# Weight chunks split between a softmax and its user, output copies moved forward in their slots, and the splits of the next tile's x moved: one edit of an attention and two-FFN kernel

## The reference, cut to what matters

```python
def _attn_ref(q, k, v):                      # 4 batches, 8 heads, 576 positions, 64 wide
    q_d, k_d, v_d = (means over groups of 4 positions)
    out_up = np.repeat(sm_attn(q_d, k_d, v_d), 4, axis=2)
    scores = np.where(abs(i - j) < 4, scale * q @ k.T, -1e9)
    return out_up + softmax(scores) @ v

x = attention.transpose(0, 2, 1, 3).reshape(2304, 512)
h = x @ w_in                                  # 512 -> 2048
x = (np.maximum(h, 0) + alpha * np.minimum(h, 0)) @ w_out
h = x @ w2_in
out = np.where(h > 0, h, np.exp(np.minimum(h, 0)) - 1) @ w2_out
```

## Time and profile before

| | us |
|---|---|
| median of 3 runs | 931.96 (930.35 to 935.31) |
| the profiled execution | 933.14 |
| its span in the trace | 931.3 |
| PE busy | 911.6 (98%) |
| DVE busy | 544.0 (58%) |
| ACT busy | 339.2 (36%) |
| POOL busy | 280.7 (30%) |
| mean granted TensorE clock | 0.993 |

### The profile page before, as it was taken

How to read it: one execution, slowest core, us unless ns; L and a number is a source line. 1 busy time by engine, 2 the same in 40 slices (tenths; PEclk the granted TensorE clock), 3 DMA queues, 4 the chain that set the end, 5 groups by cost and what they waited for, 6 DMA issues and landing times.

```text
span 931.3 us, 15268 instructions
## 1 busy us (share of the span) xinstructions
PE 911.6 (98%) x5616; PEld 851.6 (91%) x5616; DVE 544.0 (58%) x1071; ACT 339.2 (36%) x784; POOL 280.7 (30%) x399
## 2 busy tenths in 40 slices
PE   8797999999999999999999999999999999999998
PEld 6697999999999999999999998888888898888887
DVE  6663566655665555454456475656765657756563
ACT  6762444444443332232232132323442234523233
POOL 3799872111111125554656541110011100000000
PEclk9998999999999999999999999999999999999999
DMA  7655531222111123353444234333453443544411
GB/s 168 147 149 147 129 110 41 54 54 51 49 45 28 29 61 125 122 161 125 159 152 143 68 125 123 113 116 113 124 181 115 115 123 114 170 126 122 115 46 69
DMA packets 119834, 100.70 MB, mean 108 GB/s; under 512 B 66000, under 2 KB 82384, under 8 KB 119760
## 3 DMA queue, kind: packets, MB, share of 16 engines
q1 hardware_dynamic: 118576, 99.42, 37.5%
q10 hardware_dynamic: 1184, 0.30, 0.2%
HBM read 80.29 MB, written 19.40 MB: 107 GB/s over the span
## 4 chain that ended last, share of the span: by engine, by line
PE 88%; POOL 6%; DVE 3%; issue 2%; ACT 1%; DVEq 0%; POOLq 0%; ACTq 0%
PE ps L243 27%; PE ps L245 26%; PE ps L244 26%; PE ps L442 2%; POOL w_in_lo L731 1%; POOL w_out_lo L731 1%; PE ps L486 1%; PE ps L424 1%; POOL w_hi L723 1%; DVE common L300 1%; PE ps L432 1%; PE ps L473 1%; POOL p_l L703 1%; POOL p_c L700 1%; PE ps L457 1%
## 5 line engine op out<-in xcount | busy, mean ns | idle before, releaser
L245 PE MATMUL ps<-common,w_hi 128*128 128x384 f32 x768 | 258.8, 337 | 0.0
L244 PE MATMUL ps<-common,w_hi 128*128 128x384 f32 x768 | 258.6, 337 | 0.0
L244 PEld LDWEIGHTS ps<-common,w_hi 128*128 128x128 f32 x768 | 145.2, 189 | 0.0
L245 PEld LDWEIGHTS ps<-common,w_hi 128*128 128x128 f32 x768 | 144.8, 189 | 0.0
L243 PE MATMUL ps<-common,w_in_lo 128*128 128x384 f32 x384 | 133.9, 349 | 0.4 <-DVE common L300 0.4
L243 PE MATMUL ps<-common,w_out_lo 128*128 128x384 f32 x384 | 132.9, 346 | 0.5 <-DVE common L322 0.5
L318 ACT ACTIVATE common<-act_g 128x384 fp32r<-128x384 f32 x96 | 50.4, 525 | 214.6 <-PE ps L245 125.1
L882 ACT ACTIVATE act_g<-act_g 128x384 f32<-128x384 f32 x96 | 50.5, 526 | 196.0 <-DVE act_g L878 196.0
L243 PE MATMUL ps<-w_hi,common 128*128 128x512 f32 x288 | 113.8, 395 | 1.7 <-ACT xT L331 1.0
L307 DVE TENSOR_SCALAR act_g<-ps,alpha_t 128x384 f32<-128x384 f32 x96 | 59.2, 617 | 95.5 <-PE ps L245 95.3
L245 PE MATMUL ps<-w_hi,common 128*128 128x512 f32 x288 | 113.5, 394 | 0.0
(11 more groups left out here) (104 smaller groups left out, 1537.2 us busy)
## 6 DMA issues: line engine op xcount, KB each, us to landing
ring<-w_in_parts SPq DMA_DIRECT2D x168, 256.0 KB, 2.7
w_in_parts<-parts SPq DMA_DIRECT2D x8, 1280.0 KB, 5.7
qk_nat<-in_q SPq DMA_DIRECT2D x32, 144.0 KB, 2.8
v_nat<-in_v SPq DMA_DIRECT2D x16, 288.0 KB
out<-xT SPq DMA_DIRECT2D x18, 256.0 KB, 2.2
qk_nat<-in_k SPq DMA_DIRECT2D x30, 144.0 KB, 3.2
v_win<-in_v SPq DMA_DIRECT2D x64, 67.5 KB
xT<-in_moe_w_in SPq DMA_DIRECT2D x16, 256.0 KB, 2.9
```

The costliest lines, as they stand in the source:

```text
L244: pe.matmul(psum, l_hi, r_lo, start=False, stop=False)
L245: return pe.matmul(psum, l_hi, r_hi, start=False, stop=stop)
```

## The change

It has three parts. (1) `LATE` becomes chunks 4, 5 in the step of unit 4, then 6 to 9, 10 to 13, and 14, 15 in the steps of units 5, 6 and 7; before it was 4 to 7, 8 to 11, 12 to 15 and none. POOL and SP both follow it. (2) On ACT, the copies of slots 5 and 6 of the second FFN stand first in their slots. (3) `tile_order` takes, instead of one chunk number, a table that says behind which second product each piece of the next tile's x is split. Tiles 1 and 2: pieces 0 and 1 behind (14, 2) and (14, 3), pieces 2 and 3 behind (15, 0) and (15, 1). Tile 0: the same, but piece 3 behind (15, 3), as before. The other tiles keep their places.

```diff
-            if (what, c) == ("second", split_at):
-                for kk in range(i, KC if i == sums - 1 else i + 1):
-                    yield "split", kk
+            if what == "second" and (c, i) in splits:
+                yield "split", splits[c, i]
...
-            LATE = [range(min(BATCH_UNITS + 4 * j, FC), min(BATCH_UNITS + 4 * (j + 1), FC)) for j in range(BATCH_UNITS)]
-            assert LATE[-1].stop == FC
+            LATE = [range(BATCH_UNITS, BATCH_UNITS + 2),
+                    *(range(n, min(n + 4, FC)) for n in range(BATCH_UNITS + 2, FC, 4))]
+            assert len(LATE) == BATCH_UNITS and LATE[-1].stop == FC
...
+            Y_COPIES = {(0, 6): range(KC - 2), (1, 0): range(KC - 2, KC)}
...
+            MIXED_SPLITS = {(FC - 2, KC - 2): 0, (FC - 2, KC - 1): 1, (FC - 1, 0): 2, (FC - 1, 1): 3}
+            FIRST_TILE_SPLITS = {(FC - 2, KC - 2): 0, (FC - 2, KC - 1): 1, (FC - 1, 0): 2, (FC - 1, KC - 1): 3}
+            REST_SPLITS = {(FC - 2, kk): kk for kk in range(KC)}
...
-                        if J == 1 and p == 0:
-                            for m in (KC - 2, KC - 1):
+                        if (J, p) in Y_COPIES:
+                            for m in Y_COPIES[J, p]:
                                 copy_y(act, TILES - 1, m)
+                        if J and J % HC == 0:
+                            for k in COPIES_BEHIND.get(p, ()):
+                                copy_out(act, J // HC - 1, k)
                         if p == 0:
...
-                        if J and J % HC == 0:
-                            for k in COPIES_BEHIND.get(p, ()):
-                                copy_out(act, J // HC - 1, k)
-                        if J == 0 and p == 6:
-                            for m in range(KC - 2):
-                                copy_y(act, TILES - 1, m)
```

More of the change, by code:

```diff
@@ L125, in last_on, with tile_order @@
         return next((order[m] for m in range(n - 1, -1, -1) if bank_of(*order[m]) == bank), None)
-    def tile_order(ahead, sums, split_at, attention=(), lead=(0, 0), seconds=FC):
+    def tile_order(ahead, sums, splits, attention=(), lead=(0, 0), seconds=FC):
         early = KC - 1 if any(lead) else KC
@@ L940, in attention_then_two_ffns @@
             block = ctx.enter_context(nc.Block())
+            MIXED_SPLITS = {(FC - 2, KC - 2): 0, (FC - 2, KC - 1): 1, (FC - 1, 0): 2, (FC - 1, 1): 3}
+            FIRST_TILE_SPLITS = {(FC - 2, KC - 2): 0, (FC - 2, KC - 1): 1, (FC - 1, 0): 2, (FC - 1, KC - 1): 3}
+            REST_SPLITS = {(FC - 2, kk): kk for kk in range(KC)}
             def first_order(t):
-                return tile_order(FIRST_AHEAD, KC, FC - 1, bursts(t), (0, 0) if t else (1, 1))
+                return tile_order(FIRST_AHEAD, KC, FIRST_TILE_SPLITS if t == 0 else MIXED_SPLITS, bursts(t),
+                                  (0, 0) if t else (1, 1))
             def rest_order(t):
-                return tile_order(REST_AHEAD, KC, FC - 2, seconds=FC - REST_AHEAD if t == TILES - 1 else FC)
+                return tile_order(REST_AHEAD, KC, REST_SPLITS, seconds=FC - REST_AHEAD if t == TILES - 1 else FC)
             LAST_SECONDS = [(c, m) for c in range(FC - REST_AHEAD, FC) for m in range(KC)]
```

## The result

The changed kernel takes 921.53 us (median of 4 runs, 919.72 to 921.87) against 932.98 us for the kernel before (median of 4, 930.35 to 935.31; with one run more than in the table above). The ratio is 0.9874, 95% interval 0.9843 to 0.9905, so it is faster by 1.26%. The forecast was 921.4. The profiled execution took 921.41 us; its span is 919.6, 11.7 less than before.

What follows compares the result with a forecast made beforehand. PE bounds the kernel, busy 911.6 of 931.3 us. Gains 7.9 + 0.9 + 2.4 = 11.2 us gave 921.9 from the profiled execution, 920.8 from the median; forecast 921.4, between them, range 918.5 to 925.5.

Steps and rivals of the forecast that it cites:

- Part 1, the wait: PE before TC of unit 5: the 5.64 us wait for POOL's normalisation goes, plus 0.17 of lost matmul overlap.
- Part 1, the clock: PE from TC to TL of unit 5: the half clock behind the wait goes with it, giving back 2.05 us.
- The rival price of 5.8 for part 1: At unit 5: if the clock is not linked to the wait, only 5.8 us is won; no separate chance given.
- Part 2, the copies: Second FFN, steps 1, 9 and 17: earlier ACT copies remove PE's waits, 1.3 plus 1.1, together 2.4 us.
- the wait named for L897: Steps 9 and 17: the trace names L897, but PE waits for ACT's copy freeing bank 0; 1.1 us for two.
- Part 3, the splits: Ends of tiles 0 and 1: earlier splits of x remove PE's wait for the low part, 0.9 us for two.
- The sign that was set for it: Ends of tiles: the last low part of x should end about 2 us behind `write_x`, not 4.
- Costs taken as nothing: Moved chunks, loads, `unit_hi` and `write_x`: taken as 0; bounds up to 1.0 for splits and 1.5 for copies.
- (a): Rival: only the idle goes, or moved splits and copies eat a piece of the gain; 924 to 926.5 us, chance 0.10.
- (b): Rival at unit 5: another releaser close behind POOL stops PE; 929 us, chance 0.05 together with one stop of (c).
- (c): Rival: split weights late, PE stops at chunks 6, 10, 14, 7.9 us each; 945 us, chance 0.01 in full.

Runs made afterwards that it cites:

- filler: The kernel before with 38 matmuls more on PE, results unused, in the place of the long wait before TC of unit 5; median 929.5 us.
- late3: The changed kernel with 3, 4, 4, 1 chunks in the steps of units 4 to 7 instead of 2, 4, 4, 2; median 921.45 us.
- no_p2: The changed kernel with ACT's copies last in slots 5 and 6 again; median 923.95 us.
- no_p3: The changed kernel with tiles 0 to 2 splitting the next x in the old places, behind products (15, kk); median 922.24 us.
- late0: The changed kernel with 0, 6, 4, 2 chunks in the steps of units 4 to 7 instead of 2, 4, 4, 2; median 928.02 us.
- pool_later: The changed kernel with POOL held before unit 8's normalisation until DVE has split all of tile 1's x; 923.3 us in one run.
- no_p1: The changed kernel with the old table of chunks `LATE`; median 928.91 us.

## Why the prediction was right, point by point

- **Part 1, the wait.** Forecast 5.81, measured 5.79. POOL's dates were right to 0.2 us at chunk 6, to 0.6 at the end of chunk 9 (98.1 for 97.5), where a second load was late, and to 1 at every later chunk.
- **Part 1, the clock.** Forecast 2.05, measured 2.06, and shown to hang on the wait by `filler` (2.0 with the wait's place filled). The rule of the Trainium skill that I weighed there ("TensorE: Matmul & The Clock Gate", "What's actually happening": idle time throttles the array) agrees for the waits of 2.14 us and more; behind the 1.61 us of `late3` the clock stayed at 1.00. The rival price of 5.8 for part 1 is out.
- **Part 2, the copies.** Forecast 2.4. Between the products p = 5 (x_last) of steps 0 and 1 lie 15.01 us now, 16.28 before, so 1.27 for the copy of y; steps 8 to 9 and 16 to 17 take 15.82, before 16.38, so 0.56 each. Sum 2.4. That the wait named for L897 was really for the copy of the output is borne out: moving only copies removed it, and it came back in `no_p2`. The first copies of y now begin at 543.32, and PE's unit product starts at 545.23 with no idle time.
- **Part 3, the splits.** Forecast 0.9, measured 1.4 to 1.5 (0.54, 0.54 and 0.34 at the ends of tiles 0, 1 and 2; 818.72 - 817.26 = 1.46 by `no_p3`). Two things were off. First the mechanism of the sum: "DVE's four low parts come one after another ... because each waits for ACT" was wrong; they ran at half speed against POOL. So the three low parts didn't shrink to 0.5 each, and "the last ends ... a microsecond before PE asks" failed. It ended at 153.43, and PE's fourth product started at 153.49, 0.57 after the third, which came 0.52 after the second. The sign that was set for it failed too: the last low part ended 3.0 us behind `write_x` (150.47), not 2 (4.0 before). The gain came all the same, 0.54 in each of the two places for a forecast of 0.5 (from TC of unit 8 to 9, and of 12 to 13, 25.24 and 28.70 became 24.70 and 28.16), because the first low part is out of the way before POOL starts, which takes one slow low part off DVE's row. That this was just enough is luck: the prediction counted on a microsecond to spare, and there was none. Second, a term was missing. At the end of tile 2 PE's fourth first product was late too, before the change:

```profile
347.19 0.38 PE L243 MATMUL ps<-common,w_in_lo 128*128 128x384 f32 x1
347.92 0.45 PE L243 MATMUL ps<-common,w_in_lo 128*128 128x384 f32 x1
```

Their starts are 0.73 apart instead of 0.52, yet no idle time is drawn, because a matmul is drawn 0.34 long and the gap is shorter than that overlap. After the change no first product at that place is more than 0.52 behind the other. From unit 13's TC to the second FFN's first product the two kernels differ by 0.34 us (255.57 and 255.23), which is this term.
- **Costs taken as nothing.** The chunks, the loads in SP's order, `unit_hi` put back by 0.3 us, `write_x` put back by 0.5: none shows as a wait of PE. What the parts won in their own places, 5.79 + 2.06 + 2.39 + 0.54 + 0.54 + 0.34 = 11.66, is within 0.1 us of the sum of the three pieces, 11.63, so nothing was lost elsewhere.
- **Rivals.** (a) and (b) are out: the clock did not fall, and no second releaser stood behind POOL. (c) appeared in one of the tables tried, with chunk 4 itself behind the normalisation (`late0`); the stop then cost 6.9 us. The prediction priced a stop at 7.9.

The median agreed to 0.1 us, which is partly luck: single runs of the changed kernel lay 2 us apart (919.72 to 921.87), and the sum of the pieces was 11.6 where 11.2 was forecast.

## What to carry to other kernels

When an engine with spare time feeds two customers, look at which one has the nearer date: here POOL had chunk 6 split at 78.57, which PE used only at 98.75, while the softmax stood on the critical path, and moving work by two chunks cost nothing until a chunk was wanted at once. Price a wait of TensorE as its idle time, plus the lost overlap of one matmul (0.17 us here), plus what the clock costs if it falls behind the wait (1.4 to 2.7 us here); and look for start-to-start gaps, since a gap shorter than a matmul is drawn long is in no list of waits. Compare variants of a long kernel piece by piece between landmarks, not by medians alone.

## What the runs showed of the hardware that was not expected

- A VectorE subtraction of 128x384 elements with both inputs in SBUF took 0.51 to 0.56 us beside an idle GpSimd and 1.02 (three in 3.05) beside GpSimd's multiplications and sums; GpSimd's pair of 96x324 multiplications went from 1.42 to 1.74.
- The clock of the first 60 us differs between executions of the same instructions (0.94 and 0.77 from 30 to 60 us in the two windows above), and TC of unit 4 started anywhere from 57.2 to 62.3 us.
- A wait of 1.61 us left the clock at 1.00, and waits of 2.14 (`pool_later`) and 2.22 (`no_p1`) were followed by matmuls at 0.50; waits of 5.64 and 9.63 cost the same 2.1 us of clock, and the 4.04 us stop of `late0` 6.88 - 4.04 - 0.17 = 2.7. The price goes with how long the clock then stays at 0.50, and is about half of it: it stood at 0.50 from 83.71 to 86.70 in `no_p1` (price 1.49), from 83.95 to 88.20 before (2.06) and from 83.04 to 88.60 in `late0` (2.7). What sets that length is left open.
